# Keys split by GpSimd from transposed copies, key loads and reciprocals as whole rows, and a new order of the attention steps

## The reference

```python
q_pool = q.reshape(B, H, S // 2, 2, D).mean(axis=3)       # B 4, H 8, S 1152, D 64
scores = scale * np.matmul(q_pool, k.transpose(0, 1, 3, 2))
scores = scores - np.max(scores, axis=-1, keepdims=True)
attn = np.exp(scores)
attn = attn / (np.sum(attn, axis=-1, keepdims=True) + 1e-09)
attn_out = np.matmul(attn, v)
h = x @ w_in; g = where(h >= 1, h, where(h <= -1, 0, (h + 1) ** 2 / 4)); x = g @ w_out
y = maximum(maximum(x @ w1, x @ w2), x @ w3) @ w2_out
```

## Time and profile before

| | |
|---|---|
| median of 3 runs | 1249.55 us (1247.94 to 1249.88) |
| profiled execution | 1249.17 us, its span 1247.4 us |
| mean granted TensorE clock | 0.997 |
| busy PE, DVE, ACT, POOL | 1224.6, 751.9, 614.2, 276.3 us |
| kT<-k_split, copies of keys into place | 60 transfers, 288 KB, 5.5 us to landing |
| k_raw<-in_k, key loads | 32 transfers, 288 KB, 6.4 us to landing |

### The profile page before, as it was taken

The page is one execution under the profiler, slowest core; times in us unless marked ns, Lnnn a source line. Parts: engine busy times, 40 slices in busy tenths (PEclk is TensorE's granted clock), DMA queues, the critical chain, the costliest instruction groups (busy, mean ns, idle before and its releaser), DMA issues.

```text
span 1247.4 us, 20668 instructions
## 1 busy us (share of the span) xinstructions
PE 1224.6 (98%) x7661; PEld 1182.5 (95%) x7661; DVE 751.9 (60%) x1575; ACT 614.2 (49%) x1462; POOL 276.3 (22%) x240
## 2 busy tenths in 40 slices
PE   7999999999999999989999999999999999999998
PEld 6999999999999999889999999999999999999998
DVE  5999999999999999844444444444452232322221
ACT  5988899889988999822222222222221111111111
POOL 3133333333333333479000000000580000000000
PEclk9999999999999999999999999999999999999999
DMA  3565665666666664443100000000230000000000
GB/s 95 96 113 113 115 114 115 115 115 115 115 115 115 112 116 80 81 114 122 33 1 1 1 1 1 1 1 1 68 102 1 1 26 26 1 26 26 1 26 26
DMA packets 124610, 76.26 MB, mean 61 GB/s; under 512 B 62560, under 2 KB 111712, under 8 KB 124512
## 3 DMA queue, kind: packets, MB, share of 16 engines
q1 hardware_dynamic: 124512, 74.94, 29.4%
HBM read 47.71 MB, written 4.79 MB: 42 GB/s over the span
## 4 chain that ended last, share of the span: by engine, by line
PE 90%; DVE 3%; POOL 2%; ACT 2%; DMA 1%; SPq 1%; issue 1%; DVEq 0%; POOLq 0%; ACTq 0%
PE hid L900 32%; PE acc L928 15%; PE values L519 11%; PE trans L437 10%; PE scores L502 6%; PE scores L503 6%; PE acc L960 6%; DVE neg_max_parts L649 1%; PE trans L457 1%; PE trans L447 1%; POOL w_slots L872 1%; DVE pT_lo L663 1%; DMA q_raw<-in_moe_w_out 1%; ACT pT_hi L559 0%; ACT probs L568 0%
## 5 line engine op out<-in xcount | busy, mean ns | idle before, releaser
L649 DVE TENSOR_REDUCE neg_max_parts<-scores 128x1 f32<-128x384 f32 x432 | 227.3, 551 | 10.1 <-PE scores L503 5.8
L663 DVE TENSOR_TENSOR pT_lo<-trans,pT_hi 128x384 fp32r<-128x384 f32 x432 | 225.9, 547 | 4.1 <-ACT pT_hi L559 2.8
L559 ACT ACTIVATE pT_hi<-trans 128x384 fp32r<-128x384 f32 x432 | 206.4, 495 | 41.4 <-PE trans L437 35.8
L568 ACT ACTIVATE probs<-scores,neg_max 128x768 f32<-128x768 f32 (+1 forms) x288 | 212.9, 744 | 6.0 <-DVE neg_max L656 5.0
L437 PE MATMUL trans<-ident,probs 128*128 128x128 f32 x1296 | 200.9, 275 | 4.8 <-DVE pT_lo L663 2.3
L502 PE MATMUL scores<-kT,qT 128*128 128x384 f32 x480 | 182.1, 379 | 1.7 <-ACT probs L568 1.1
L437 PEld LDWEIGHTS trans<-ident,probs 128*128 128x128 f32 x1296 | 155.8, 140 | 20.4 <-DVE pT_lo L663 8.9
L900 PE MATMUL hid<-qT,w_slots 128*128 128x384 f32 x936 | 172.5, 338 | 2.6 <-POOL w_slots L872 2.6
L900 PEld LDWEIGHTS hid<-qT,w_slots 128*128 128x128 f32 x936 | 164.3, 189 | 3.8 <-POOL w_slots L872 2.9
L900 PE MATMUL hid<-x_hi,w_slots 128*128 128x384 f32 x624 | 167.6, 335 | 0.0
L503 PE MATMUL scores<-kT,qT 128*128 128x384 f32 x480 | 162.3, 338 | 0.0
(11 more groups left out here) (99 smaller groups left out, 1781.0 us busy)
## 6 DMA issues: line engine op xcount, KB each, us to landing
kT<-k_split SPq DMA_DIRECT2D x60, 288.0 KB, 5.5
k_raw<-in_k SPq DMA_DIRECT2D x32, 288.0 KB, 6.4
v_raw<-in_v SPq DMA_DIRECT2D x32, 288.0 KB
q_raw<-in_q SPq DMA_DIRECT2D x32, 256.0 KB, 3.3
k_split<-value_all SPq DMA_DIRECT2D x64, 72.0 KB, 2.8
out<-X SPq DMA_DIRECT2D x18, 256.0 KB, 2.8
q_raw<-in_moe_w_out SPq DMA_DIRECT2D x14, 256.0 KB, 3.1
k_raw<-in_moe_w SPq DMA_DIRECT2D x12, 256.0 KB, 3.2
```

Source lines behind the costliest of these rows:

```text
L559: act.activation(*tile_places(pT[0], src, s % TILES, g), ACT.Copy).then_inc(p_hi_done, 1)
L568: act.activation(probs[:, par, :].rearrange("p (n k) -> p n k", n=GROUPS)[:, ns[0]:ns[-1] + 1], scores[:, bank:bank + len(ns), 0:SB], ACT. ...
L649: dve.tensor_reduce(neg_max_parts[:, par, n:n + 1], scores[:, score_banks(s)[n], 0:SB], AX_X, ALU.max, negate=True).then_inc(parts_done, 1)
L663: dve.tensor_tensor(*tile_places(pT[1], src, s % TILES, g), hi.bitcast(F32), ALU.subtract).then_inc(p_lo_done, 1)
```

## The change

Four things are changed.

- **Key load**: one transfer a pair, in which each partition gets two whole rows of 2304 B (one for each head); before it was two transfers of 128 x 9 pieces of 256 B. Since the heads now stand one behind the other, a transposed block of 128 columns holds two key blocks of one head, and of the 9 blocks one is shared; `KEY_BLOCKS` tells the value products the new order of the blocks.
- **Key split**: ScalarE copies the transposed keys unrounded over the raw ones (`k_turned` is the same memory as k_raw). When all three groups are there, GpSimd rounds them into k_parts and subtracts for the rest, two instructions over 1152 columns, in its new step `keys(i + 1)`, behind the values of head 1. VectorE's key step is gone. `place_k` waits for GpSimd and copies in six transfers instead of four (same bytes).
- **Reciprocals**: a new step R on TensorE transposes the 128 x 9 reciprocals, ScalarE keeps them, and SyncE sends nine rows of 512 B; before, 128 x 9 single values.
- **Order**: all three tables are new. VectorE's has no K, its R stands behind L0.0.

```diff
@@ orders: the row of tile 7 in each @@
 PE_ORDER
-T7.0 V1:11-18 T7.1 S9.0 T7.2 S9.1 S9.2
+T7.0 T7.1 V1:11-15 S9.0 V1:15-18 T7.2 S9.1
 ACT_ORDER
-H7.0 E8.0 H7.1 V1 H7.2 E8.1
+H7.0 H7.1 E8.0 H7.2 E8.1 V1
@@ sp_program @@
         def load_k(pair):
-            for h in range(2):
-                src = k_heads[bass.ds(head(pair) + h, 1)].rearrange("h p (t d) -> p (h t) d", d=D)
-                sp.dma_start(k_raw[:, :, h, :], src).then_inc(k_loaded, 16)
+            src = k_pairs[bass.ds(head(pair) // 2, 1)].rearrange("c p h n -> p (c h) n")
+            sp.dma_start(k_raw.rearrange("p h t d -> p h (t d)"), src).then_inc(k_loaded, 16)
...
-            sp.wait_ge(k_lo_done, pair * KG)
-            for h in range(2):
-                for a in range(2):
-                    copy_parts(sp, kT[rows_of(a), pair % 2, h, :], k_parts[rows_of(h), a, :], k_placed)
+            sp.wait_ge(k_split_done, pair)
+            places = kT[:, pair % 2].rearrange("p h s -> p (h s)")
+            for a in range(2):
+                copy_parts(sp, places[rows_of(a), ODD:ODD + S], k_parts[rows_of(0), a, :], k_placed)
+                copy_parts(sp, places[rows_of(a), 0:ODD], k_parts[rows_of(1), a, 0:ODD], k_placed)
+                copy_parts(sp, places[rows_of(a), ODD + S:2 * S], k_parts[rows_of(1), a, ODD:S], k_placed)
 
         def send_recips(pair):
 
-            sp.wait_ge(recip_done, pair + 1)
-            sp.dma_start(recip_rows[pair % 2].rearrange("(t p) -> p t", p=P), recips[:],
-                         allow_slow_non_contiguous=True).then_inc(recip_sent, 16)
+            sp.wait_ge(recip_kept, pair + 1)
+            sp.dma_start(recip_rows[pair % 2].rearrange("(t p) -> t p", p=P), recips_turned[:]).then_inc(recip_sent, 16)
@@ pool_program @@
+        def keys(pair):
+
+            pool.wait_ge(k_kept, pair * KG)
+            if pair >= 2:
+                pool.wait_ge(k_placed, 96 * (pair - 1))
+            pool.sem_inc(passed, 1)
+            pool.tensor_scalar(k_parts[:, 0, :], k_turned, 1.0, 0.0, ALU.mult, ALU.add).then_inc(k_rounded, 1)
+            pool.wait_ge(k_rounded, pair)
+            pool.tensor_tensor(k_parts[:, 1, :], k_turned, k_parts[:, 0, :].bitcast(F32), ALU.subtract
+                               ).then_inc(k_split_done, 1)
...
             head_values(i, 1)
+            if i + 1 < PAIRS:
+                keys(i + 1)
             if i > 0:
-                add_values(i - 1, 3, (v_ready, 2 * i + 2))
+                add_values(i - 1, 3, (k_split_done, i + 1) if i + 1 < PAIRS else (v_ready, 2 * i + 2))
                 scale(i - 1)
@@ pe_program @@
+        def recip_transposes(pair):
+
+            group = ("R", pair, 0)
+            wait_bank(group)
+            pe.wait_ge(recip_done, pair + 1)
+            pe.transpose(trans[0:TILES, BANK[group], 0:P], recips[:], ident[:]).then_inc(recip_trans_done, 1)
@@ act_program @@
         def keys(pair, g):
 
             act.wait_ge(k_trans_done, (pair - 1) * KG + g + 1)
-            act.activation(k_parts[:, 0, g * GK * P:(g + 1) * GK * P], trans[:, BANK["K", pair, g], 0:GK * P],
-                           ACT.Copy).then_inc(k_hi_done, 1)
+            act.activation(k_turned[:, g * GK * P:(g + 1) * GK * P], trans[:, BANK["K", pair, g], 0:GK * P],
+                           ACT.Copy).then_inc(k_kept, 1)
...
+        def keep_recips(pair):
+
+            act.wait_ge(recip_trans_done, pair + 1)
+            if pair > 0:
+                act.wait_ge(recip_sent, 16 * pair)
+            act.activation(recips_turned[:], trans[0:TILES, BANK["R", pair, 0], 0:P], ACT.Copy).then_inc(recip_kept, 1)
@@ dve_program @@
-        def keys(pair, g):
-
-            dve.wait_ge(k_hi_done, (pair - 1) * KG + g + 1)
-            cols = slice(g * GK * P, (g + 1) * GK * P)
-            dve.tensor_tensor(k_parts[:, 1, cols], trans[:, BANK["K", pair, g], 0:GK * P],
-                              k_parts[:, 0, cols].bitcast(F32), ALU.subtract).then_inc(k_lo_done, 1)
```

More of the change, by code:

```diff
@@ L53 @@
 K0
-H0.0 E1.0 E1.1 H0.1 W2 H0.2 K1 E2.0 E2.1
-H1.0 H1.1 H1.2 E3.0
-H2.0 E3.1 H2.1 K2 H2.2
-H3.0 E4.0 H3.1 W3 E4.1 H3.2 Q0
-H4.0 E5.0 H4.1 Q1 E5.1 H4.2
-H5.0 E6.0 E6.1 H5.1 V0 H5.2
-H6.0 E7.0 Q2 E7.1 H6.1 H6.2
-H7.0 E8.0 H7.1 V1 H7.2 E8.1
-H8.0 H8.1 E9.0 E9.1 H8.2
+H0.0 H0.1 E1.0 K1 E1.1 H0.2 W2
+H1.0 E2.0 H1.1 R E2.1 H1.2
+H2.0 H2.1 E3.0 H2.2 E3.1 K2
+H3.0 H3.1 E4.0 H3.2 W3 Q0 E4.1
+H4.0 H4.1 E5.0 H4.2 E5.1 Q1
+H5.0 H5.1 E6.0 E6.1 V0 H5.2
+H6.0 H6.1 E7.0 Q2 H6.2 E7.1
+H7.0 H7.1 E8.0 H7.2 E8.1 V1
+H8.0 H8.1 H8.2 E9.0 E9.1
 """
 DVE_ORDER = """
-K0 R
-L0.0 M2.0 M2.1 M2.2 L0.1 M3.0 L0.2 K1 M3.1 M3.2
-L1.0 L1.1 L1.2 M4.1
-L2.0 M4.2 L2.1 M4.0 K2 L2.2 M5.0
-L3.0 L3.1 M5.1 M5.2 L3.2 Q0
-L4.0 M6.0 L4.1 M6.1 M6.2 Q1 L4.2 M7.1
-L5.0 M7.2 M7.0 L5.1 L5.2
-L6.0 M8.0 Q2 M8.1 M8.2 L6.1 L6.2
-L7.0 M9.0 L7.1 M9.1 M9.2 L7.2 M10.1
-L8.0 L8.1 M10.2 M10.0 L8.2
+L0.0 R L0.1 M2.0 M2.1 M2.2 L0.2
+L1.0 M3.0 L1.1 M3.1 M3.2 L1.2
+L2.0 L2.1 M4.1 L2.2 M4.2 M4.0
+L3.0 M5.0 L3.1 L3.2 M5.1 M5.2 Q0
+L4.0 L4.1 M6.0 L4.2 M6.1 M6.2 Q1
+L5.0 L5.1 M7.1 M7.2 M7.0 L5.2
+L6.0 L6.1 M8.0 Q2 M8.1 M8.2 L6.2
+L7.0 M9.0 L7.1 L7.2 M9.1 M9.2
+L8.0 L8.1 M10.1 L8.2 M10.2 M10.0
 """
@@ L111, in sb @@
         return memory.enter_context(nc.sbuf_tensor(name, shape, dt))
-    k_raw = shared["k_raw"][:].rearrange("p (t h d) -> p t h d", t=KT, h=2)
+    k_raw = shared["k_raw"][:].rearrange("p (h t d) -> p h t d", h=2, t=KT)
+    k_turned = shared["k_raw"][:]
+    KEY_BLOCKS = [*range(1, KT, 2), *range(0, KT, 2)]
+    ODD = KT // 2 * P
     q_raw = shared["q_raw"][:].rearrange("p (t n) -> p t n", t=TILES)
@@ L184, in ring_order @@
                     groups.append((step[0], pair + 1, step[1]))
-        return groups
+                elif step[0] == "R" and pair > 0:
+                    groups.append(("R", pair - 1, 0))
+        return groups + [("R", PAIRS - 1, 0)]
     _groups = ring_order()
@@ L443, in key_transposes @@
             wait_bank(group)
-            pe.wait_ge(k_loaded, 32 * (pair + 1))
+            pe.wait_ge(k_loaded, 16 * (pair + 1))
+            rows = k_raw.rearrange("p h t d -> p (h t d)")
             for j in range(GK):
-                src = k_raw[:, g * GK + j].rearrange("p h d -> p (h d)")
+                src = rows[:, (g * GK + j) * P:(g * GK + j + 1) * P]
                 last = pe.transpose(trans[:, BANK[group], j * P:(j + 1) * P], src, ident[:])
@@ L481, in tile_scores @@
             if first and t == 0 and pair > 0:
-                pe.wait_ge(k_placed, 64 * pair)
+                pe.wait_ge(k_placed, 96 * pair)
                 pe.wait_ge(q_lo_done, pair * QG)
@@ L518, in value_products @@
                     pe.wait_ge((p_hi_done, p_lo_done)[part], (pair * TILES + t + 1) * GROUPS)
-                last = pe.matmul(values[:, 0:HALF], v_split[:, h, kt].rearrange("p a d -> p (a d)"),
+                last = pe.matmul(values[:, 0:HALF], v_split[:, h, KEY_BLOCKS[kt]].rearrange("p a d -> p (a d)"),
                                  pT[part][:, h, kt, half * HALF:(half + 1) * HALF],
@@ L550, in pe_program @@
                     query_transposes(pair + 1, step[1])
+                elif kind == "R" and pair > 0:
+                    recip_transposes(pair - 1)
         for step in steps_of(PE_ORDER):
@@ L637, in act_program @@
                     queries(pair + 1, step[1])
+                elif kind == "R" and pair > 0:
+                    keep_recips(pair - 1)
         meanwhile()
@@ L641, in act_program @@
                 keep_values(PAIRS - 1, step[1])
+        keep_recips(PAIRS - 1)
     def dve_program(dve, meanwhile):
@@ L709, in reciprocals @@
             if pair > 0:
-                dve.wait_ge(recip_sent, 16 * pair)
+                dve.wait_ge(recip_trans_done, pair)
             par = pair % 2
@@ L739, in dve_program @@
                     tile_max(pair * TILES + step[1], step[2])
-                elif kind == "K" and pair + 1 < PAIRS:
-                    keys(pair + 1, step[1])
                 elif kind == "Q" and pair + 1 < PAIRS:
@@ L922, in second1 @@
                 pe.wait_ge(*ends["values_kept"])
+                pe.wait_ge(*ends["recips_kept"])
             elif f == 0:
```

42 lines of the change are left out of this document (24 added, 18 removed).

## The result

| | before | after |
|---|---|---|
| median | 1249.69 us (1247.94 to 1249.88, 4 runs) | 1308.13 us (1301.87 to 1310.72, 4 runs) |
| ratio | | 1.0465 (95% interval 1.0445 to 1.0485) |
| span of the profiled execution | 1247.4 us | 1300.1 us |
| mean granted TensorE clock | 0.997 | 0.989 |

The account below looks back on a forecast made before the run. TensorE was taken as the bound, losing 1.3 us a pair mostly because VectorE frees banks late. Fourteen pairs 3.7 us longer: 1247.4 + 51.8 - 5.1 = 1294.1 us of span, 1296 us forecast, range 1262 to 1328.

Parts of the forecast that it names:

- The way of the keys: GpSimd's value split, key split, then six copies: copies issued 21.1 us into the pair, keys in place at 29.1.
- W3: TensorE's products for value part 3 of the pair before, which GpSimd's value split waits for: done at 14.5 us.
- The add of part 2: GpSimd's add of value part 2, behind the reciprocals on the queue: at about 13 us into the pair, not 15.
- The first wait: TensorE waits for the key copies before the next pair's first scores: it arrives 2.4 us too early.
- S9.0: TensorE's first scores of the next pair, which wait for the key copies: reached at 26.7 us with waits.
- V2: TensorE's value part that needs ScalarE's keep of value part 1: reached at 32.2 us, done at 35.3.
- the second wait: TensorE waits before V2 for ScalarE's keep of value part 1, held by the late add of part 3: 1.8 us.
- The queue behind them: SyncE's queue behind the key copies: 11.5 us from first copy to the add of part 3, between 10.1 and 12.7.
- The key load: 590 KB in whole rows on SyncE's queue: 2.0 us against 3.0 in 256-byte pieces; it mends neither wait.
- The edges: Start, first and last pair, and the weight wait after the attention: together 5.1 us gained.
- TensorE's floor: A pair's TensorE work summed from pitches: 30.7 us, leaving 1.3 us of 31.98 lost in small waits.
- the order hides it: Rival: keys in place by S9.0, so TensorE decides; 31.1 us a pair, 1232 us; chance 0.10.

Follow-up runs that it names:

- h_after_again: The changed kernel, unchanged, run again on another chip against the kernel before: 1305.91 us, ratio 1.0265.
- b_move_ahead: The changed kernel with SyncE issuing the reciprocals' spread and the move of value part 3 ahead of the key copies: 1265.73 us, ratio 0.9946.
- c_fill: b_move_ahead with 14 idle identity transposes on TensorE ahead of its wait for the key copies: 1267.53 us, ratio 0.9966.
- a_keys_first: The changed kernel with GpSimd splitting the keys ahead of the second head's values: 1240.43 us, ratio 0.9755; on another chip 1242.11 us, 0.9759.
- f_key_rows: The kernel before with only the whole-row key load, its block order and six copies: 1269.03 us, ratio 0.9977.
- k_single_values: a_keys_first with the reciprocals sent as 1152 single values again, the transposes and ScalarE's copy still made: 1389.43 us, ratio 1.0925.

## Why the prediction was right, and where it was off

**The way of the keys held.** The copies are issued 21.2 us into the pair (21.1 predicted), but two errors cancel in that. W3's last product begins at 14.6 and its record ends at 15.0, where I had 14.5; and the key split took 3.9 us (323.61 to 327.53) where 4.2 was scaled from half its columns: in both instructions twice the short one is 0.19 us more than the long one. The add of part 2 comes at 11.8 us (predicted near 13), VectorE is at 324 of 400 us, 81% (81%).

**The first wait was mis-sized, without effect on the pair.** S9.0 waited 1.2 us, not 2.4. I took 8.0 us for the copies, and in this pair the last of them was there 7.4 after the first issue: the keys were in place at 28.7, not 29.1. The larger part is TensorE's own way, which I had too short: it reached S9.0 at 27.5 us, not 26.7. From there to V2 it took 3.4 instead of 3.1, and so it came to V2 at 32.1, as predicted (32.2), because the shorter wait and the longer way cancelled; that was luck. In pairs 1 to 5 the copies took 8.6 to 9.1 us and S9.0 waited 2.4 to 2.9. The pair doesn't follow that, since the second wait ends at the same place: where S9.0 comes earlier, V2 waits longer. In h_after_again a pair with copies of 8.6 us and full clock takes 35.3.

**The queue behind them held.** From the first copy to the add 327.55 to 339.08, 11.5 us (11.5); V2's wait 2.0 (1.8), up to 34.1 (34.0). The pair at full clock 35.6 (35.7). This is the term on which the pair ends, and b_move_ahead shows it: the same copies without it give 33.1.

**The key load** took 5.6 us to landing for both heads' 576 KB; before, each half of it took 6.4 (median). Among the DMA issues of the changed kernel:

```profile
k_raw<-in_k SPq DMA_DIRECT2D x16, 576.0 KB, 5.6
```

The direction is the one that the Trainium skill gives (DMA: Bandwidth & Descriptors, Why small descriptors are slow (HBM only)). The gain is at the start of the kernel; in the pairs the queue's 11.5 us contain it, and it mended neither wait, as predicted.

**The clock was not in the sum.** I had only counted waits, as at full speed. In the attention the trace has seven stretches at clock 0.50, 27 us in all; each begins during one of the two waits or at most 1.6 us behind it. The eight pairs with 1.7 us or more of such a stretch take 36.6 to 37.8 us, the five others 35.4 to 35.7. Over the thirteen pairs the mean is 36.48: 0.9 a pair above 35.6, some 11 us. TensorE's busy time for the same instructions is 33.07 us a pair on average against 32.27 at full clock, 10 us in the thirteen, so the clock is nearly all of it. This is read from the trace; c_fill, which was to test it, didn't.

**The edges were worth more.** Predicted 5.1; the start and the first pair gave 3.1 for 2.0, and behind the fifteenth K0 the change is -2.6 where the terms gave +0.6 (one more waiting pair, less 0.5 and 2.6). The wait for the weight went, and the stretch at half clock behind it too, which I had not counted. So +10.4 in the pairs, -1.1 and -3.2 at the edges: 1294.1 becomes 1300.1. The median lay 6 above the profiled execution.

**TensorE's floor was wrong, without harm here.** The pitches gave 30.7 us and "1.3 us of small waits". The trace of before has a pair in which TensorE doesn't wait at all:

```profile
276.57:307.99 31.42, 31.42 (x232) 30.28 (x231) 30.12 (x72) 28.41 (x73) 10.91 (x11) 1.00 0.65 115
```

It takes 31.42 us, so only some 0.55 of the 31.98 was waiting. The other 0.7 I take for time at the switches between transposes and matmuls, which pitches taken inside long stretches leave out; that is argued, not shown. It would also explain that TensorE came late to S9.0. VectorE's freed 1.5 us could bring that little and no more. By a floor of 31.6 the rival "the order hides it" would have read about 1240 instead of 1232, which is what a_keys_first then took. That rival named its own condition rightly: W3 must not be the last one, and moving two lines lifts it.

## What to carry to other kernels

When work moves to an engine with spare time, look at what stands ahead of its place there: GpSimd had 65% free, but behind the step that waits for W3 the 3.9 us made a pair 3.6 us longer than before, and ahead of it no longer at all. Count every step that stands behind on the same DMA queue too, since the second wait, on which the pair ends, came from there. Look at what stands ahead on that queue as well: one slow transfer there moves everything behind it. And take an engine's floor from a stretch in which it never waits, not from pitches.

## What the runs showed of the hardware

- 1152 values of 4 bytes on SyncE's queue hold back what stands behind them: a move issued 1.3 us later reached its add 12.9 us after its issue (304.37 to 317.24), behind nine rows of 512 B 2.9 us (280.42 to 283.32).
- ScalarE, which is not on that queue, stalls 9.6 to 12.5 us behind the issue of such single values: twelve times and four times in the kernel before on two chips, seven times in f_key_rows, nine in k_single_values on a third chip, for 0.7 to 3.2 us. In the ten traces of kernels that send rows there is no such stall. Why is open.
- The kernel before took 1249.7 us on one chip and 1270.8 to 1273.2 on four others, the changed one 1308.1 and 1305.9, a_keys_first 1240.4 and 1242.1. On the one of the four whose trace of the kernel before was read, what stands behind the single values comes some 2 us later and the stalls are longer; why is open.
- The granted clock fell to 0.50 during or up to 1.6 us behind waits of only 1.8 to 2.9 us, seven times in the attention of the changed kernel; with one wait of 1.2 to 3.0 us a pair (b_move_ahead) once in fourteen pairs, and with one of 4.6 to 7.0 us (k_single_values) in every pair.
- The same six copies took 7.4 us in most pairs and 8.6 to 9.1 in five of the same execution. Why is open too.
